# First batch of an attention, gated MLP and Fourier kernel: four input buffers, a split first transfer and another order of steps

## The reference, cut to what matters

```python
# 1: linear attention with decays, a state of 48 x 48 for each head
state = alpha[:, :, t, :, None] * state + einsum('bhd,bhe->bhde', k[:, :, t], v[:, :, t])
y[:, :, t] = einsum('bhd,bhde->bhe', q[:, :, t], state)
# 2: gated MLP; u and v are the halves of gelu(x @ w_in), 512 wide each
v_n = layer_norm(v) * g_ln
v_s = einsum('ts,bsd->btd', w_sg, v_n) + b_sg[None, :, None]
x1 = x + (u * v_s) @ w_out
# 3: Fourier mixing and a second MLP
u = x1 + real(fft(fft(x1, axis=1), axis=2))
out = u + relu(layer_norm(u) @ w_ch1) @ w_ch2
```

## Time and profile before

| | us |
|---|---|
| median of 3 runs | 788.97 (788.46 to 790.69) |
| profiled execution: its time | 788.8 |
| profiled execution: its span | 787.0 |
| PE busy, DVE busy, ACT busy in the span | 746.0, 465.9, 194.6 |
| 0 to 50 us: PE busy, DVE busy | 30.05, 33.81 |
| 50 to 100 us: PE busy, DVE busy | 48.63, 40.44 |
| 100 to 160 us: PE busy, DVE busy | 59.23, 43.63 |
| PE idle for DVE's `kd` of chunk 2, for `x_lo` (0 to 104 us) | 4.1, 3.5 |
| issue to landing: values of chunks 1 to 5; a chunk's `akq` later on (median) | 13.8; 5.2 |

### The profile page before, as it was taken

The page is one execution under the profiler, slowest core; times in us unless marked ns, Lnnn a source line. Parts: engine busy times, 40 slices in busy tenths (PEclk is TensorE's granted clock), DMA queues, the critical chain, the costliest instruction groups (busy, mean ns, idle before and its releaser), DMA issues.

```text
span 787.0 us, 12141 instructions
## 1 busy us (share of the span) xinstructions
PE 746.0 (95%) x4900; PEld 723.0 (92%) x4900; DVE 465.9 (59%) x1015; ACT 194.6 (25%) x366; POOL 75.3 (10%) x123
## 2 busy tenths in 40 slices
PE   4779999999999999999996699999999999999997
PEld 4668899989999899999996699999999999999997
DVE  5787877689675978747656763537263534432121
ACT  1212521133111331124223242123212232112111
POOL 1011100011000210014004112000210010000000
PEclk9889999999999999999999799999999999999999
DMA  7432322321312231215228021201220010000000
GB/s 228 142 95 79 98 80 55 111 76 46 91 46 76 76 91 47 76 64 161 81 74 268 11 61 36 66 1 34 78 82 1 30 60 0 30 4 27 1 31 31
DMA packets 20986, 54.02 MB, mean 69 GB/s; under 512 B 2484, under 2 KB 14792, under 8 KB 20936
## 3 DMA queue, kind: packets, MB, share of 16 engines
q1 hardware_dynamic: 17416, 42.52, 17.8%
q0 software_dynamic: 2816, 9.10, 3.8%
q10 hardware_dynamic: 704, 1.71, 0.7%
HBM read 43.86 MB, written 9.46 MB: 68 GB/s over the span
## 4 chain that ended last, share of the span: by engine, by line
PE 87%; DVE 6%; DMA 4%; issue 1%; ACT 1%; POOL 0%; DVEq 0%; SPq 0%
PE bank L1039 73%; PE bank L1090 4%; DMA decay_k_q<-in_akq 3%; PE bank L1065 3%; PE bank L1086 2%; PE bank L1078 2%; PE bank L1221 1%; PE bank L1055 1%; PE bank L1111 1%; DVE u_kept L1000 1%; PE bank L1045 1%; DMA u_new<-x_scratch,mirrored_rows 1%; DVE fwd L795 1%; DVE rev L781 1%; DVE w_in_lo L767 0%
## 5 line engine op out<-in xcount | busy, mean ns | idle before, releaser
L1039 PE MATMUL bank<-ut_hi,w_c_parts 128*128 128x384 f32 x576 | 163.9, 340 | 1.3 <-DVE ut_lo L977 1.3
L991 DVE SCALAR_TENSOR_TENSOR hidden_lo<-bank,hidden_hi 128x384 fp32r<-128x384 f32 x96 | 53.3, 555 | 126.5 <-ACT hidden_hi L714 125.4
L1039 PEld LDWEIGHTS bank<-ut_hi,w_c_parts 128*128 128x128 f32 x576 | 105.6, 188 | 1.5 <-issue 1.5
L1039 PE MATMUL bank<-w_c_hi,hidden_hi 128*128 128x384 f32 x288 | 97.1, 337 | 0.7 <-DVE u_kept L1000 0.7
L1039 PE MATMUL bank<-w_c_lo,hidden_hi 128*128 128x384 f32 x288 | 96.7, 336 | 0.0
L1039 PE MATMUL bank<-w_c_hi,hidden_lo 128*128 128x384 f32 x288 | 96.7, 336 | 0.0
L1039 PE MATMUL bank<-ut_lo,w_c_parts 128*128 128x384 f32 x288 | 96.5, 335 | 0.0
L714 ACT ACTIVATE hidden_hi<-bank 128x384 fp32r<-128x384 f32 x96 | 47.3, 492 | 199.2 <-PE bank L1039 199.2
L1039 PE MATMUL bank<-w_sg_hi,vn_hi 128*128 128x384 f32 x192 | 66.1, 344 | 0.7 <-ACT u_gelu L647 0.7
L1039 PE MATMUL bank<-w_sg_hi,vn_lo 128*128 128x384 f32 x192 | 64.2, 335 | 0.0
L1039 PE MATMUL bank<-w_sg_lo,vn_hi 128*128 128x384 f32 x192 | 64.2, 334 | 0.0
(11 more groups left out here) (167 smaller groups left out, 1493.8 us busy)
## 6 DMA issues: line engine op xcount, KB each, us to landing
decay_k_q<-in_akq SPq DMA_DIRECT2D x21, 672.0 KB, 5.2
x_scratch<-x_half SPq DMA_DIRECT2D x8, 579.0 KB, 3.6
out_tiles<-u_kept SPq DMA_DIRECT2D x24, 192.0 KB, 2.0
values<-in_v SPq DMA_DIRECT2D x18, 192.0 KB, 5.2
x_quarters<-x_scratch SPq DMA_DIRECT2D x16, 168.9 KB
raw_weights_b<-in_w_second SPq DMA_DIRECT2D x3, 768.0 KB, 4.2
u_new<-x_scratch SPq DMA_DIRECT2D x4, 576.0 KB
decay_k_q_b<-in_akq SPq DMA_DIRECT2D x3, 672.0 KB, 8.4
```

The lines of the kernel that those rows point to most:

```text
L991: nc.vector.scalar_tensor_tensor(out=hid[1][:, i % 4, :], in0=HB[i % 2][:, 0:HS], scalar=0.0, in1=f32(hid[0][:, i % 4, :]), op0=ALU.max, o ...
L1039: ins = nc.tensor.matmul(dst, a, c, start=start and n == 0, stop=stop and n == len(passes) - 1)
```

## The change

- The inputs of batch 0's chunks have four buffers (`raw_first`); the load of chunk c waits for the query of chunk c-3 only as far as `need(sp, qk_done, c - 3)` says, so chunks 1, 2 and 3 are issued at the start without a wait.
- The decays of chunk 0 (224 KB) are a transfer of their own on SP with the semaphore `alpha_in`; its keys and queries (448 KB) are ACT's first transfer, before the three tables, of which `blk` is now the last. DVE waits for the keys only before `kd`.
- SP issues the first two weight pieces behind chunk 3, and pieces 2, 3, 4 and 5 all before `P1_FIRST`.
- `FIRST_DVE`, `FIRST_PE` and a new `FIRST_ACT` hold all u and v products and all splits of batch 0; the products go over four banks (`first_bank`), each waiting for the GELU that emptied its bank.
- `P1_FIRST` holds no u product, no split and no v tail any more; its s steps start one chunk earlier.
- `WARM_SCORES` has 24 fillers instead of 40.

```diff
-WARM_SCORES = {0: 8, **{c: 8 for c in range(2, NT)}}
+WARM_SCORES = {0: 6, 1: 4, 2: 8, 3: 6}
...
+FIRST_DVE = ([("prep", 0), ("query", 0), ("prep", 1), ("query", 1), ("scores", 0), ("prep", 2)]
+             + [("scores", 1), ("out", 0), ("carry", 1), ("query", 2), ("prep", 3)]
+             + [("scores", 2), ("out", 1), ("carry", 2), ("query", 3), ("split", 0), ("prep", 4), ("x", 0)]
+             + [("scores", 3), ("out", 2), ("carry", 3), ("query", 4), ("split", 1), ("prep", 5), ("x", 1)]
+             + [("scores", 4), ("out", 3), ("carry", 4), ("query", 5), ("x", 2), ("next prep", 0)]
+             + [("scores", 5), ("out", 4), ("carry", 5), ("x", 3), ("v", 0), ("next query", 0), ("x", 4), ("x", 5)]
+             + [("v", 1), ("split", 2), ("next scores", 0), ("v", 2), ("split", 3), ("v", 3), ("split", 4), ("v", 4)]
+             + [("split", 5), ("v", 5), ("v end", 0), ("v end", 1)])
...
+FIRST_PE = ([("scores", 0), ("scores", 1), ("out", 0), ("scores", 2), ("out", 1), ("x", 0), ("scores", 3), ("out", 2)]
+            + [("x", 1), ("scores", 4), ("out", 3), ("x", 2), ("v", 0), ("scores", 5), ("u", 0), ("out", 4), ("x", 3)]
+            + [("u", 2), ("out", 5), ("x", 4), ("u", 4), ("x", 5), ("u", 6), ("v", 1), ("u", 1), ("next scores", 0)]
+            + [("u", 3), ("v", 2), ("u", 5), ("v", 3), ("u", 7), ("v", 4), ("v", 5)])
+FIRST_PRODUCTS = [step for step in FIRST_PE if step[0] in ("u", "v")]
+FIRST_ROLLED = FIRST_PRODUCTS.index(("u", 4))
+FIRST_U = [i for step, i in FIRST_PRODUCTS if step == "u"]
...
+P1_FIRST = ([("load", 1), ("prep", 1), ("out", 0), ("carry", 1), ("query", 1), ("s", 0), ("scores", 1)]
+            + [("load", 2), ("s", 1), ("prep", 2), ("out", 1), ("carry", 2), ("query", 2), ("s", 2), ("scores", 2)]
+            + [("load", 3), ("prep", 3), ("out", 2), ("carry", 3), ("query", 3), ("s", 3), ("scores", 3)]
+            + [("load", 4), ("s", 4), ("prep", 4), ("out", 3), ("carry", 4), ("query", 4), ("s", 5), ("scores", 4)]
+            + [("load", 5), ("prep", 5), ("out", 4), ("carry", 5), ("query", 5), ("s", 6), ("load", NT), ("s", 7)]
+            + [("scores", 5), ("end", 0), ("next x", 0), ("next x", 1), ("out", 5)])
...
+        raw_first = [set_a["raw"], set_b["raw"], place("decay_k_q_c", [PR, 3, G, P], F32, at_yn),
+                     place("decay_k_q_d", [PR, 3, G, P], F32, at)]
...
+        def first_bank(step, i):
+
+            at = FIRST_PRODUCTS.index((step, i))
+            slot = max(at - FIRST_ROLLED, 0) % 4
+            before = [k for k in range(at) if max(k - FIRST_ROLLED, 0) % 4 == slot]
+            return bank[(4, 0, 1, 2)[slot]], FIRST_PRODUCTS[before[-1]] if before else None
...
             def load_first(c):
-                need(sp, qk_done, c - 1)
-                sp.dma_start((set_a, set_b)[c % 2]["raw"][:].rearrange("p a g t -> p (a g t)"),
-                             akq[c]).then_inc(akq_in[c % 2], 16)
-
-            for c in range(NT):
+                need(sp, qk_done, c - 3)
+                sp.dma_start(raw_first[c % 4][:].rearrange("p a g t -> p (a g t)"), akq[c]).then_inc(akq_in[c % 4], 16)
+
+            sp.dma_start(set_a["raw"][:, 0].rearrange("p g t -> p (g t)"), akq[0][:, 0:G * P]).then_inc(alpha_in, 16)
+            for c in range(1, 4):
                 load_first(c)
-                if c == 3:
-                    load_piece(sp, 2)
+            load_piece(sp, 0)
+            load_piece(sp, 1)
+            load_first(4)
+            load_first(5)
+            load_piece(sp, 2)
             load_piece(sp, 3)
+            load_chunk(1, 0)
             load_piece(sp, 4)
-            load_chunk(1, 0)
+            load_piece(sp, 5)
...
-            for dst, src in ((blk, blk_in), (ident, ident_in), (mask, mask_in)):
+            act.dma_start(set_a["raw"][:, 1:3].rearrange("p a g t -> p (a g t)"),
+                          akq[0][:, G * P:3 * G * P]).then_inc(akq_in[0], 16)
+            for dst, src in ((ident, ident_in), (mask, mask_in), (blk, blk_in)):
                 act.dma_start(dst[:], src).then_inc(masks_in, 16)
...
+                    if i == 0:
+                        dve.wait_ge(akq_in[0], 16)
                     nc.vector.tensor_tensor(kd[:], raw[:, 1], rev[:], ALU.mult).then_inc(kd_done, 1)
...
+            def wait_first_bank(step, i):
+                before = first_bank(step, i)[1]
+                if before is not None and before[0] == "v":
+                    pe.wait_ge(vg_done, before[1] + 1)
+                if before is not None and before[0] == "u":
+                    pe.wait_ge(ug_done, FIRST_U.index(before[1]) + 1)
+                if FIRST_PRODUCTS.index((step, i)) > FIRST_ROLLED:
+                    pe.wait_ge(yn_done, NT)
+                    pe.wait_ge(sm_done, 2 * NT)
```

More of the change, by code:

```diff
@@ new lines @@
+FIRST_ACT = ([("scores", 0), ("scores", 1), ("out", 0), ("scores", 2), ("out", 1), ("split", 0), ("x", 0), ("scores", 3)]
+             + [("split", 1), ("out", 2), ("x", 1), ("scores", 4), ("out", 3), ("x", 2), ("v", 0), ("scores", 5)]
[3 rows of a table added]
+FIRST_PE = ([("scores", 0), ("scores", 1), ("out", 0), ("scores", 2), ("out", 1), ("x", 0), ("scores", 3), ("out", 2)]
[3 rows of a table added]
+FIRST_PRODUCTS = [step for step in FIRST_PE if step[0] in ("u", "v")]
+FIRST_ROLLED = FIRST_PRODUCTS.index(("u", 4))
+FIRST_U = [i for step, i in FIRST_PRODUCTS if step == "u"]
@@ L659, in phase1 @@
                         first_products(b, step, i)
-                    elif step in ("u", "v tail"):
-                        if step == "u":
-                            gate(b, i)
+                    elif step == "u":
+                        gate(b, i)
                         if i in (2, 3):
                             vn_hi(b, NT - 4 + i)
-                        if isinstance(b, int) and b == 0 and (step, i) in SPLIT_IN_FIRST:
-                            split_hi(SPLIT_IN_FIRST[step, i])
                     elif step == "s":
@@ L723, in _ @@
             act.wait_ge(masks_in, 48)
[L724 to L727, removed]
+            for step, c in FIRST_ACT:
+                if step == "split":
                     split_hi(c)
@@ L735, in _ @@
                 elif step in ("x", "v"):
-                    if (step, c) == ("x", NT - 1):
-                        attend(0, "out", c, *first_set(c)[:2])
                     first_products(0, step, c)
+                elif step == "v end":
+                    vn_hi(0, NT - 2 + c)
             for b in range(B):
@@ L1010, in _ @@
                     dve.wait_ge(masks_in, 48)
-                if step == "split lo":
+                if step == "split":
                     split_lo(c)
@@ L1129, in gate @@
                 f, h = i // 2, i % 2
[L1130 to L1134, removed]
+                if isinstance(b, int) and b == 0:
+                    wait_first_bank("u", i)
+                    pe.wait_ge(xlo_done, HT * (h + 1))
+                    pe.wait_ge(w_lo_done, 2)
                 elif i < 5:
```

55 lines of the change are left out of this document (31 added, 24 removed), and 3 rows, old and new, of the table FIRST_ACT.

## The result

The changed kernel takes 790.46 us (median of 20 runs, 789.01 to 794.21), the kernel before 788.71 us (20 runs too): a ratio of 1.0028, interval 1.0017 to 1.0038. It is 1.7 us slower where 3.4 us less were forecast.

The account below looks back on a forecast made before the run. Masks, then VectorE's list, were taken to bound the start, later TensorE's work and VectorE's tail: 21.9 + 70.8 + 63.7 = 156.4 us against 159.75, 3.4 less, so 785.5 us, range 780.5 to 790.5.

Parts of the forecast that it names:

- the opening: Start transfers: first decays at about 6.5 us, masks at 15.5 against 10.07, VectorE's preparation of chunk 2 at 21.9 against 22.28.
- that sum: Bytes moved before the masks land in the opening: 2.5, 0.6 and 0.2 MB, given as 3.2 MB, 11.7 us at 273 GB/s.
- A: Time when VectorE starts preparing chunk 2, forecast at 21.9 us; later steps of batch 0 are counted from it.
- Rivals 1 and 3: Opening: masks at 11 us, ACT's queue in lots, 780.8 us, chance 0.17; masks at 21 behind SP's queue, 791.1, 0.08.
- TensorE from query 5: Batch 0's products: v 0 from A+28.9 to A+31.1, hidden by VectorE, later no gap, v 2 done at A+55.1.
- a rival with a chance of 0.14 and the number 792.1: Clock falls in TensorE's gaps between A+18.6 and A+28.8, slowing v 0, u 0, u 2, scores: 6.6 us, 792.1 us, chance 0.14.
- The point of comparison: First transpose for batch 1, after which both kernels run the same orders: forecast at 156.4 us against 159.75.
- the tail: VectorE's steps after v 2 (GELU, v steps, splits, low halves): 14.6 us in the list, last low half at A + 70.8.
- the wait before the spatial product: TensorE idle before batch 0's first spatial product, until VectorE's last low half is done: 3.5 us.
- Rival 4: Front's idle time returns before the first spatial product and batch 1's chunk 1, VectorE steps 3 us longer: 789 us, chance 0.11.

Follow-up runs that it names:

- e1: Changed kernel with 8 fillers put back for chunk 4 (32 in all): 788.00 us, ratio 0.9984 to the kernel before.
- e5: Changed kernel's transfers with the step lists, product banks and 40 fillers of the kernel before: 782.94 us, ratio 0.9943 to the kernel before.
- e6: Changed kernel with a third staging buffer and v products 1 to 5 ahead of u products 6, 1, 3, 5, 7: 787.69 us, ratio 0.9995 to the kernel before.
- e2: Changed kernel with chunk 0's keys and queries on SP behind the decays, only tables on ACT's queue: 785.89 us, ratio 0.9969 to the kernel before.
- e9: e10 with chunk 0's keys and queries on SP, as in e2: 781.43 us, ratio 0.9899 to the kernel before.
- e10: e5 without the fillers of chunks 4 and 5 (24 left), masks still late: 785.78 us, ratio 0.9957 to the kernel before.
- e4: Kernel before with only the changed kernel's 24 fillers for its 40: 785.76 us, ratio 0.9961 to the kernel before.
- e12: e9 with 8 fillers put back for chunk 5 (32 in all): 775.86 us, ratio 0.9845 to the kernel before.
- e7: Changed kernel with e1, e2 and e6 in one: 779.49 us, ratio 0.9897 to the kernel before.
- e11: e9 with chunk 0 in one transfer of 672 KB on SP: 783.60 us, ratio 0.9915 to the kernel before.

## Why the prediction was wrong

**Right: the opening.** The masks were forecast for 15.5 us and came at 14.85; chunk 2 was forecast for 21.9 and was prepared from 21.27. The first decays came earlier than I said (VectorE starts at 5.15, not 6.5), but this was lost in the wait for the masks, as forecast. The bytes in that sum make 3.3 MB and not 3.2, which would have given 15.8. For batch 0's later chunks VectorE waited for no transfer, and its list ran as forecast up to query 4 (done at 43.8 us, A+22.5). The Trainium skill's page "DMA: Bandwidth & Descriptors" ("Queues, rings and completion order") says that an engine empties a packet, typically of 9 to 17 descriptors, before it changes the ring. This case doesn't show it: the landings of 7.7, 10.1 and 12.4 us for three chunks and 8.3, 10.9 and 12.7 for three tables went in step. The landings alone would also fit turns by whole transfers of 7 or 8 rows for each engine, but the counts don't: from 10.0 to 10.5 us SP's queue moved 25 descriptors and ACT's 27, as in the earlier trace rows. Rivals 1 and 3 are out.

**The step that failed: "TensorE from query 5", v 0 at A+28.9 for 2.17 us.** It started at A+31.8 and took 3.9 us. The premise one paragraph earlier, that the fillers taken out "cost and bring nothing here except through the clock", was right, and the clock then was priced as a rival with a chance of 0.14 and the number 792.1. That rival is what happened, at the gap that it named as the longest (2.3 us forecast, 2.00 measured), but it was off at both ends. It left out 3 at its price, and out 3, mostly matmuls of 48 and 96 columns, took nearly twice its time (45.95 to 52.6 us, 6.7 instead of 3.5). It doubled u 0 and u 2, and u 0 ran at the full clock (58.56 to 60.23 us, 1.7). So its price of 6.6 us, and with it 792.1, was too high: e1 gave back 3.5. What misled me was the reading of the earlier trace rows against the whole idle time of 4.1 us: TensorE's last work before that row ended at 20.44 us, so the row was itself proof that the clock was down 2 us later. The argument for the safe side ("work lies between the gaps") had no row behind it.

**How the steps add up.** The point of comparison was forecast for 156.4 us and came at 161.84, 5.4 later. Chunk 2's preparation began 0.6 earlier, v 2 ended 4.8 later relative to it (A+59.9 instead of A+55.1), the tail took 1.0 more and the rest 0.2. The failed step is nearly all of it.

**Mis-sized: the tail.** From v 2's end to the last `vn_lo` 15.7 us were forecast and 16.7 measured; the wait before the spatial product was 4.88 instead of 3.5. The 1.0 has several small parts: VectorE waited 0.8 us for the last piece's split instead of 0.5, the last two low halves took 1.5 instead of 1.2, and the steps of v 3 to v 5 a little more each. The wait grew by 1.4 us: these 1.0, and TensorE needed 11.9 us instead of 12.2 from v 2's end to it. New was that the clock falls in this wait too (0.50 from 95 us), so that the first spatial product takes 4.7 us and not 3.2. From there to the transpose for batch 1 63.9 us were measured (97.92 to 161.84), 63.7 forecast: the slow product took up most of the time in which TensorE would have waited for the next query.

**Rival 4.** Its sign, the spatial product after 96 us, came (97.92), but mostly through the clock: VectorE's steps in the tail were 1.0 us longer together, not 3. A wait that I had not listed, of batch 1's `kd` for scores 5 (2.66 us), appeared only with the low clock; e1 doesn't have it. It is part of the failed step.

**The sum by experiments.** By the ratios: four buffers and the other transfers with late masks -4.5 us (e5), the new order with 24 fillers +6.7. Of the latter, 3.5 are the clock around chunk 4 (e1) and 2.6 the tail (e6). The late masks, 4.7 us (e2; 4.6 in the old order, e9 against e10), stand against a gain of the transfers of some 9 us. With the clock held up the changed kernel is at 787.4 us (e1, by its ratio), 1.9 over the forecast: 1.0 of it is the longer tail, the rest isn't assigned.

## What to carry to other kernels

A dummy matmul can be plain work on TensorE's path (e4) or what keeps its clock up (e1, e12): before cutting one, find the idle time that it fills, and after each change elsewhere look where the idle time has moved (in the old order chunks 4 and 5 needed none, with the new transfers chunk 5 did, in the new order chunk 4). Whatever shares a semaphore with the first instruction should go ahead of bulk data on its queue, however small it is: two DMA queues here took turns by rows, so a table of 0.9 KB landed 1.8 us behind the one before it, nearly as far as the 672 KB chunk beside it behind its own (2.3). When work is moved forward to fill one idle stretch, ask what it had been covering where it was.

## What the runs showed of the hardware that was not expected

- An idle time of 2.0 to 2.2 us of TensorE was enough for its clock to fall from 2.4 to 1.2 GHz: at 43.2 us, while it idled (the changed kernel), or at 54.2 us, 1.6 us after it was back at work (e9). In e7 it fell in an idle time of 1.25 us, which in e1 it did not.
- The clock then stayed low for 12.9 us of unbroken work in the changed kernel (to 56.8 us), of which the first 9.2 were matmuls of 48 to 128 columns and the rest of 512; in e7, with matmuls of 512 columns from 47.2 us on, only from 46.0 to 49.4 us. 16 filler records in the idle time kept the clock up in e1 and e12. Where 2.1 us were left idle (e9, e10, e11), the runs of one kernel lie in two groups some 5.5 us apart.
- At the lower clock an attention output with 48 and 96 columns takes 6.7 us instead of 3.5.
- The semaphore of the tables was complete at 14.85 to 16.3 us in six executions with the same opening, and at 9.3 to 11.8 in five with the keys on SP: the same opening varies by 1.5 to 2.5 us from one profiled execution to another, as much as the change moved the time or more.
